# Gate columns copied sooner, chunk 2 spread ahead of chunk 0's values, output gates and weight splits in another order, in a linear-attention and gated-feed-forward kernel on one core

## What is computed

```python
for t in range(S):
    m_new = np.maximum(f_gate[:, :, t] + m, i_gate[:, :, t])
    f_stab = np.exp(f_gate[:, :, t] + m - m_new)
    i_stab = np.exp(i_gate[:, :, t] - m_new)
    m = m_new
    C = f_stab[:, :, None, None] * C + i_stab[:, :, None, None] * np.einsum('bhd,bhe->bhde', vt, kt)
    n = f_stab[:, :, None] * n + i_stab[:, :, None] * kt
    denom = np.maximum(np.abs(np.einsum('bhd,bhd->bh', n, qt)), 1.0)[:, :, None]
    y[:, :, t] = sigmoid(o_gate[:, :, t]) * np.einsum('bhde,bhe->bhd', C, qt) / denom
x = (sigmoid(x @ w_gate) * (x @ w_val)) @ w_out
x = ((x @ w_a) * (x @ w_b)) @ w_out2
```

## Time and profile before

| | |
|---|---|
| median of the runs | 471.15 us |
| the profiled execution's own time | 470.95 us |
| its span | 468.9 us |
| PE busy | 458.4 us (98%), 2527 matmuls |
| DVE, ACT, POOL busy | 190.2, 197.4, 114.4 us |
| granted TensorE clock | 1.00 of full speed over the whole span |
| transfers | 37.42 MB, mean 80 GB/s |

### The profile page before, as it was taken

One profiled execution on the slowest core, in us unless ns is written; L12 is line 12 of the kernel. 1 busy time (PEld: TensorE's weight loads), 2 busy tenths in 40 slices (PEclk: granted clock), 3 DMA queues, 4 the chain that ended last, 5 costly groups with the idle time before them and its releaser, 6 DMA issues.

```text
span 468.9 us, 6630 instructions
## 1 busy us (share of the span) xinstructions
PE 458.4 (98%) x2527; PEld 403.5 (86%) x2527; DVE 190.2 (41%) x352; ACT 197.4 (42%) x360; POOL 114.4 (24%) x110
## 2 busy tenths in 40 slices
PE   8898999999999999999999999999999999999997
PEld 5787898898989898888888888888888888888886
DVE  7866346546564636334222243222232222322223
ACT  5863829574573828224344352222222222222222
POOL 4487746664032020002444541000000000000000
PEclk9999999999999999999999999999999999999999
DMA  5886764842524362000333200000010000100001
GB/s 146 226 240 197 235 192 131 251 130 75 159 83 125 113 183 93 1 2 0 100 122 111 98 0 1 0 2 0 1 56 1 0 1 0 58 0 1 0 1 56
DMA packets 21449, 37.42 MB, mean 80 GB/s; under 512 B 2835, under 2 KB 15670, under 8 KB 21418
## 3 DMA queue, kind: packets, MB, share of 16 engines
q1 hardware_dynamic: 21050, 35.94, 24.9%
q10 hardware_dynamic: 208, 0.71, 0.5%
q0 software_dynamic: 160, 0.35, 0.3%
HBM read 34.91 MB, written 2.04 MB: 79 GB/s over the span
## 4 chain that ended last, share of the span: by engine, by line
PE 92%; POOL 3%; DMA 2%; DVE 1%; SPq 1%; issue 1%; ACT 0%; POOLq 0%
PE bank L573 54%; PE bank L590 27%; PE bank L497 3%; PE bank L472 2%; DMA q_blk<-kq_in 2%; PE bank L488 1%; PE bank L463 1%; DMA vk<-vk_in 1%; PE bank L553 1%; POOL w_lo L1109 1%; PE bank L523 1%; PE bank L511 1%; POOL w_lo_mid L1109 0%; POOL w_lo_end L1109 0%; PE bank L435 0%
## 5 line engine op out<-in xcount | busy, mean ns | idle before, releaser
L944 DVE TENSOR_TENSOR h_ff<-bank,s_ff 128x512 f32<-128x512 f32 x72 | 49.7, 691 | 175.5 <-PE bank L573 175.2
L573 PE MATMUL bank<-xt,w_hi 128*128 128x512 f32 x360 | 118.6, 394 | 0.5 <-issue 0.5
L742 ACT CAST h_hi<-h_ff 128x512 fp32r<-128x512 f32 x72 | 44.6, 619 | 130.2 <-DVE h_ff L944 127.1
L735 ACT ACTIVATE s_ff<-bank 128x512 f32<-128x512 f32 x72 | 43.1, 598 | 124.1 <-PE bank L573 123.7
L573 PE MATMUL bank<-xt,w_lo 128*128 128x512 f32 x216 | 84.5, 391 | 0.0
L573 PEld LDWEIGHTS bank<-xt,w_hi 128*128 128x128 f32 x360 | 65.6, 188 | 12.3 <-issue 0.9
L950 DVE TENSOR_TENSOR h_lo<-h_ff,h_hi 128x512 fp32r<-128x512 f32 x72 | 52.5, 728 | 55.1 <-ACT h_hi L742 55.1
L573 PE MATMUL bank<-xt,w_hi_mid 128*128 128x512 f32 x180 | 59.3, 394 | 0.0
L573 PE MATMUL bank<-xt,w_hi_end 128*128 128x512 f32 x180 | 59.1, 393 | 0.0
L573 PEld LDWEIGHTS bank<-xt,w_lo 128*128 128x128 f32 x216 | 40.6, 188 | 8.8
L590 PE MATMUL bank<-w_hi,h_hi 128*128 128x320 f32 x144 | 45.1, 313 | 0.0
(11 more groups left out here) (125 smaller groups left out, 678.6 us busy)
## 6 DMA issues: line engine op xcount, KB each, us to landing
w_raw<-w_in SPq DMA_DIRECT2D x24, 544.0 KB, 3.8
vk<-vk_in SPq DMA_DIRECT2D x12, 344.0 KB, 3.6
levels<-a_scratch SPq DMA_DIRECT2D x7, 512.0 KB
k_both<-kq_in SPq DMA_DIRECT2D x18, 120.0 KB
q_blk<-kq_in SPq DMA_DIRECT2D x18, 120.0 KB
y<-rows_t SPq DMA_DIRECT2D x12, 160.0 KB, 1.9
q<-kq_in SPq DMA_DIRECT2D x10, 180.0 KB
osig_b<-o_in SPq DMA_DIRECT2D x8, 160.0 KB, 3.2
```

Of the source, the lines that this page charges most:

```text
L573: mm = pe.matmul(up_bank(u, gv)[:, :], w_part(low, f, (gv * 3 + kt) * P, P), xt[:, xb * TOK + g * TG:xb * TOK + (g + 1) * TG], start=(j == ...
L735: act.activation(s_ff[u % 2][:, :], up_bank(u, 0)[:, :], ACT.Sigmoid if u < UNITS // 2 else ACT.Copy).then_inc(act_s, 1)
L742: act.copy(h_hi[u % 2][:, :], h_ff[u % 2][:, :]).then_inc(act_h, 1)
L944: dve.tensor_tensor(h_ff[u % 2][:, :], up_bank(u, 1)[:, :], s_ff[u % 2][:, :], ALU.mult).then_inc(dve_h, 1)
```

## The change

On PE, chunk 2's spread goes ahead of chunk 0's values, the gate columns of chunks 2 and 3 are transposed before the second half of chunk 0's scores, and turn(3) goes ahead of to_state(3). ACT copies these columns between the two halves of chunk 0's weights, issues the load of osig_a one half later, and computes its sigmoid behind all of i_rows. SP loads the values of chunks 0 and 1 behind the rows of chunk 1, and chunk 2's queries ahead of the store of i_rows. POOL weighs chunk 1's values and makes low_rows before it issues chunk 3's transfers; it splits the first 384 columns of tile 0 (before: 768) ahead of open_x(3), and the rest ahead of the decays; up(0, 1) waits for that rest. Tiles 2, 5, 6, 9 and 10 are split earlier in their units, or in earlier units.

```diff
-        PARTS = ((0, 1, bank[3]), (1, 2, XY[0]), (2, CHUNKS, bank[2]))
+        PARTS = ((0, 1, bank[3]), (1, 2, bank[3]), (2, CHUNKS, bank[2]))
...
 (SP)        load_rows(0)
-            load_v(0)
             sp.wait_ge(tri_set1, 1)
             load_rows(1)
+            load_v(0)
+            load_v(1)
             sp.wait_ge(dve_split, 4)
             load_rows(2)
+            load_q(2)
             sp.wait_ge(act_irow, 1)
             store_rows(f_row, i_dram, 1, 2, st_irow)
-            load_q(2)
-            load_v(1)
...
 (PE: scores)
-                    wait(pe, act_cols, 2 if half else 0)
+                    wait(pe, act_cols, 4 if half else 0)
...
 (PE: up)
+                if u == 0 and gv:
+                    pe.wait_ge(pool_wlo, 1)
...
 (PE)        columns(0, 0, dve_gate, 5)
-            scores(0, 1)
             columns(0, 1, dve_rows, 1)
             pe.wait_ge(pool_sel, 5)
             spread(0)
+            pe.wait_ge(act_cols, 2)
+            columns(1, 0, dve_gate, 9)
+            columns(1, 1, dve_rows, 2)
+            scores(0, 1)
             scores(1, 0)
             scores(1, 1)
             spread(1)
-            pe.wait_ge(act_e, 1)
-            columns(1, 0, dve_gate, 9)
-            columns(1, 1, dve_rows, 2)
+            spread(2)
             values(0)
             to_state(0)
-            spread(2)
...
             scores(4, 0)
+            turn(3)
             to_state(3)
-            turn(3)
             scores(4, 1)
...
 (ACT)       weigh(0, 0)
+            gate_cols(1)
             weigh(0, 1)
+            weigh(1, 0)
             act.dma_start(osig_a[:, :], o_in[:, 0:ALONE * DM]).then_inc(ld_oa, 16)
-            weigh(1, 0)
             weigh(1, 1)
-            gate_cols(1)
-            act.wait_ge(ld_oa, 16)
-            act.activation(osig_a[:, :], osig_a[:, :], ACT.Sigmoid).then_inc(act_o, 1)
             act.wait_ge(act_cols, 3)
             weigh(2, 0)
             weigh(2, 1)
             for c in range(2, CHUNKS):
                 i_rows(c)
+            act.wait_ge(ld_oa, 16)
+            act.activation(osig_a[:, :], osig_a[:, :], ACT.Sigmoid).then_inc(act_o, 1)
             weigh(3, 0)
...
-            W_AT = {0: (2,), 1: (3, 4), 3: (5,), 4: (6, 7), 6: (8, 9), 7: (10, 11)}
+            W_EARLY = {0: (2,), 3: (5, 6), 6: (9, 10)}
+            W_AT = {1: (3, 4), 4: (7, 8), 7: (11,)}
...
                 gate(u)
+                for f in W_EARLY.get(u, ()):
+                    w_high(f)
...
 (POOL: w_low)
-                at = W1C if j == 0 else 0
+                at = W1C // 2 if j == 0 else 0
...
             weigh_v(0)
+            weigh_v(1)
+            (low_rows: a memset and four affine_selects, moved here)
             pool.wait_ge(pe_s, 4)
             (four dma_starts of chunk 3's keys and queries)
-            weigh_v(1)
...
             pool.wait_ge(act_whi, 1)
-            pool.tensor_tensor(w_part(1, 0, 0, W1C), w_raw[0][:, 0:W1C], w_part(0, 0, 0, W1C).bitcast(F32), ...)
+            pool.tensor_tensor(w_part(1, 0, 0, W1C // 2), w_raw[0][:, 0:W1C // 2], ...)
             open_x(3)
+            w_low(0)
             pool.wait_ge(act_dec, 1)
             decay(2)
             decay(3)
-            w_low(0)
             scale_q(4)
             pool.wait_ge(act_cols, 6)
             weigh_v(4)
             w_low(1)
-            (low_rows)
-            W_AT = {0: (2,), 1: (3, 4), 3: (5,), 4: (6, 7), 6: (8, 9), 7: (10, 11)}
+            w_low(2)
+            W_EARLY = {3: (5, 6), 6: (9, 10)}
+            W_AT = {1: (3,), 2: (4,), 4: (7,), 5: (8,), 7: (11,)}
...
                         weigh_v(n)
+                for f in W_EARLY.get(u, ()):
+                    w_low(f)
                 if k == 1 and last_with_state(n):
                     decay(n)
```

More of the change, by code:

```diff
@@ L1141, in _ @@
             weigh_v(0)
+            weigh_v(1)
+            pool.memset(low_rows[:, :], 1.0).then_inc(pool_low, 1)
+            pool.wait_ge(pool_low, 1)
+            for x in range(2):
+                pool.affine_select(low_rows[:, x:x + 1], low_rows[:, x:x + 1], [[0, 1]], ALU.is_gt, 0.0,
+                                   base=1 - (x + 1) * HD, channel_multiplier=1).then_inc(pool_low, 1)
+            pool.wait_ge(pool_low, 3)
+            for x in range(2):
+                pool.affine_select(low_rows[:, x:x + 1], low_rows[:, x:x + 1], [[0, 1]], ALU.is_gt, 0.0,
+                                   base=(x + 2) * HD, channel_multiplier=-1).then_inc(pool_low, 1)
             pool.wait_ge(pe_s, 4)
@@ L1157, in _ @@
             pool.wait_ge(act_whi, 1)
-            pool.tensor_tensor(w_part(1, 0, 0, W1C), w_raw[0][:, 0:W1C], w_part(0, 0, 0, W1C).bitcast(F32),
-                               ALU.subtract).then_inc(pool_wup, 1)
+            pool.tensor_tensor(w_part(1, 0, 0, W1C // 2), w_raw[0][:, 0:W1C // 2],
+                               w_part(0, 0, 0, W1C // 2).bitcast(F32), ALU.subtract).then_inc(pool_wup, 1)
             open_x(3)
+            w_low(0)
             pool.wait_ge(act_dec, 1)
@@ L1168, in _ @@
             w_low(1)
-            pool.memset(low_rows[:, :], 1.0).then_inc(pool_low, 1)
-            pool.wait_ge(pool_low, 1)
-            for x in range(2):
-                pool.affine_select(low_rows[:, x:x + 1], low_rows[:, x:x + 1], [[0, 1]], ALU.is_gt, 0.0,
-                                   base=1 - (x + 1) * HD, channel_multiplier=1).then_inc(pool_low, 1)
-            pool.wait_ge(pool_low, 3)
-            for x in range(2):
-                pool.affine_select(low_rows[:, x:x + 1], low_rows[:, x:x + 1], [[0, 1]], ALU.is_gt, 0.0,
-                                   base=(x + 2) * HD, channel_multiplier=-1).then_inc(pool_low, 1)
-            W_AT = {0: (2,), 1: (3, 4), 3: (5,), 4: (6, 7), 6: (8, 9), 7: (10, 11)}
+            w_low(2)
+            W_EARLY = {3: (5, 6), 6: (9, 10)}
+            W_AT = {1: (3,), 2: (4,), 4: (7,), 5: (8,), 7: (11,)}
             for u in range(3 * (NCH - ALONE) - 1):
```

## The result

The changed kernel takes 468.66 us (median of 20 runs, 467.60 to 477.68), the kernel before 472.70 (20 runs beside them, 470.74 to 480.57). The ratio of comparable runs is 0.9940 with a 95% interval of 0.9917 to 0.9963: a gain that can be measured, inside 2%. The profiled execution has a span of 466.1 us (its time 467.95) against 468.9: 2.8 us won, where the working forecast 3.55. Runs of one kernel differ by up to 10 us, a good part of it with the mean granted clock of TensorE, so beside the ratios I set the spans, and the runs with a mean clock of at least 0.999 ("clocked runs": 467.60 to 471.68 us for the changed kernel, so they too spread), against each other.

What follows compares the result with a forecast made beforehand. PE bounds the kernel, busy 458.45 of 468.90 us, with 5.92 us of waits as the ceiling. Gains of 0.8 + 1.9 + 0.85 = 3.55 us take 471.15 to 467.6 us; 8 in 10: 466.0 to 470.1.

Steps and rivals of the forecast that it cites:

- the front: Everything up to the first up-projection: gate columns, spread(2), loads, sigmoid, turn(3); start at 33.5 instead of 34.26, 0.8 us won.
- the signs put down: Expected in the trace: scores(2,0) near 14.5, wait before spread(3) at 20.5, up-projection 33.5, turn(4) 44.2, turn(6) 87.
- sign of being wrong: A wait over a microsecond behind the first up-projection, or that up-projection starting outside 32.3 to 35 us.
- the landing of chunk 3's rows: Before spread(3): last row issued at 17.2 us, landing taken as 3.3 us, so spread(3) at 20.5, 0.5 us won.
- rival B: Row loads land in 2.1 us, spread(3) waits for nothing else, turn(6) is fully covered: 466.4 us; chance 0.15.
- Rival C: Transfers eat the front: chunk 3's rows land at 22.1 or later, losing 1.1 to 1.3 us: 469.3; chance 0.20.
- Turn(4): PE's 1.99 us wait before turn(4) goes but for 0.1, as POOL splits tile 2 without idle: 1.9 us won.
- Turn(6): PE's 1.04 us wait before turn(6) shrinks, as POOL's splits of tiles 9 and 10 start earlier: 0.85 us won.
- rival D: At unit 6 tile 10 lands after 81.1 us and delays turn(6), making the kernel slower than before; chance 0.05.
- Free items: Small moves priced at nothing, among them gate_cols, the wait of up(0,1), and POOL's transfers behind weigh_v(1) and low_rows.
- rival E: Small new waits, at state_sum(2) or x_n behind longer POOL work, eat most of the gain: 470.4 us; chance 0.08.
- parts 2 and 3: The gains at turn(4), 1.9 us, and at turn(6), 0.85 us, from earlier low_rows and weight splits.

Runs made afterwards that it cites:

- Experiment 5: Changed kernel with osig_a's load issued earlier again and ACT's sigmoid of it back between chunks 1 and 2; ratio 0.9965 to the kernel before.
- 12: Second execution of the changed kernel with later chunks' i_rows moved on ACT from ahead of the sigmoid to behind x_high(0); 468.69 us, span 466.7.
- Experiment 3: Changed kernel with DVE's `sign` moved from ahead of the feed-forward loop to behind state(0), where POOL runs no split; ratio 0.9913 to the kernel before.
- 11: Kernel before with only low_rows made early on POOL, behind weigh_v(1), and `sign` left in place; ratio 0.9988 to the kernel before.
- experiment 9: Changed kernel with `sign` early behind state(0) and tile 10 split later in unit 6; ratio 0.9890 to the kernel before.
- Experiment 4: Changed kernel with tile 10 copied by ACT at the end of unit 6 and split by POOL behind open_x(6); ratio 0.9908 to the kernel before.
- experiment 6: Changed kernel with SP's loads back in the order of the kernel before, POOL's order as changed; ratio 1.0023 to the kernel before.
- kernel 10: Changed kernel with SP's loads in the old order and POOL's weigh_v(1) back behind chunk 3's transfers; ratio 0.9988 to the kernel before.
- kernel 1: Changed kernel with its front kept but low_rows, weight splits and the wait of up(0, 1) as before; ratio 0.9997 to the kernel before.
- kernel 8: Changed kernel with `sign` early, tile 10 split later and later chunks' i_rows moved behind x_high(0); ratio 0.9890 to the kernel before.

## Why the prediction was right, step by step

The time (467.6 forecast, 468.66 median, 467.95 in the profiled execution) and the bound were right: the gain is PE's idle time under a ceiling of 5.92 us, 2.8 us of it where the sum has 3.55. The sizes were off in opposite directions, the front 0.58 us better and the two turns together 1.38 us worse; that the total came this close is partly luck. Of the signs put down, scores(2,0) came as told (14.62, no wait) and neither sign of being wrong appeared; but spread(3) came at 19.00 instead of 20.5, with no wait of 1 to 2 us, and the waits before turn(4) and turn(6) are over 0.3. (A slip in the sum: 33.5 + 10.67 is 44.17, not 44.15.)

**The front: +0.8 forecast, +1.38 measured.** Issues came within 0.6 us of the working. The term that was mis-sized is the landing of chunk 3's rows: from 16.63 to spread(3) at 19.00 is at most 2.4 us, where I took 3.3; the bound from below, 2.1, was nearer. That was rival B's first half. Rival C, that the rows wait behind 344 KB of values, did not occur, but the rule cited for it was not put to the test: POOL had the values of chunk 1 at 10.46, 6 us before these rows were issued. Experiment 5 has rows issued half a microsecond behind 640 KB; they reached PE 4.0 us after issue (9.20 to 13.24), where in the changed kernel they took at most 2.5 (8.88 to spread(2) by 11.4). That is the direction of C, though not a proof of the rule. But spread(3) 2 us sooner brought only 1.4 at the up-projection, because ACT binds from there, as forecast: exp at 21.38 (forecast 20.9; 21.55 before), DVE's product of chunk 3 waits 1.76 us for it, and turn(1) waits 0.31 us for DVE and starts at 25.32, 1.39 us sooner than before (26.71). Experiment 5 prices the sigmoid's move at 0.6 to 0.9; 12 shows that ACT alone made sooner gives nothing, because the rows then set spread(3). The reverse, the rows alone sooner, was not run. The exp table cost 1.28 us and its neighbours followed at once (20.09 + 1.28 = 21.37), in agreement with the row, not with the 2.66 us of the Trainium skill (ScalarE: Activation LUTs, "What ACT_TABLE_LOAD costs").

**Turn(4): +1.9 forecast, +0.92 beyond the front.** The step that failed is "w_low(2) follows w_low(1) without idle: 39.1 + 2.5 + decay 0.76 + x_n 1.43 = 43.8". POOL did its part: its two splits ended at 41.08, where the sum has 41.6. Not in the sum was DVE. I had `sign` down as waiting for low_rows; with low_rows early it has its input, and then takes 2.47 us beside POOL's split, not 0.16. That, and h_low(0) held by the second split, made combine(4) late (x_raw at 42.18), POOL idle for 0.94 and the decay 1.19 instead of 0.76. By an estimate in the forecast's own terms POOL would have ended at 41.08 + 0.76 + 1.43 = 43.3 without them, and PE came at 43.85: no wait. Experiment 3, which moves `sign` and nothing else, takes the wait away; 11 shows the same hold on `sign` with nothing but low_rows moved. How much is lost is a matter of timing (experiment 9). The row was there to be read: `sign` of the kernel before took 0.70 us for 240 numbers.

**Turn(6): +0.85 forecast, +0.45.** Tile 10 was issued at 75.91 and reached ACT at 80.97, inside the 79.7 to 81.2 of rival D, just under the 81.1 from which it decides. ACT waited 1.12 us for it all the same with h_high(6) behind it, and h_low(6) met POOL's split of tile 10 and took 2.49 us. Experiment 4 gives the 0.47 back. But D's own sum does not give the wait: 80.97 + 5.8 = 86.8, and PE came at 87.38. x_n was done at 87.79, one microsecond later than that sum, because the decay took 1.20 us instead of 0.76 and POOL then waited 0.57 us for x_raw, which DVE made late. The step that failed is of the same kind as at turn(4): "Now w_low(9) and (10) go ahead of decay(6)" is priced on POOL alone. Whether tile 10's landing or the second split put h_low(6) where it is held, experiment 4 leaves open.

**Free items.** The wait of up(0, 1), gate_cols(0) and (1), and the five small instructions of low_rows cost PE nothing by themselves: none of them is named in PE's waits. That weigh_v(1) ahead of POOL's transfers costs nothing holds only with load_v(1) early, as the forecast assumed without saying so (experiment 6: 7.88 us of POOL). Nearest in kind was rival E, something small that eats into parts 2 and 3, for 1.4 us (2.75 forecast, 1.37 measured) and not 2.8; but of the causes it names neither was it, state_sum(2) nor longer work on POOL.

## What to carry to other kernels

When work is moved ahead on one engine, walk the queue of the engine beside it too, instruction by instruction: many of those on DVE that only read and write SBUF last until the POOL instruction that they meet is done. A tiny DVE instruction that takes 0.7 or 2.5 us is the mark of it; put it where POOL is idle, and look which instruction meets the split in its stead. When a load is moved, name what in any engine's in-order queue is placed behind its consumer.

## What the runs showed of the hardware

**POOL holds DVE.** A 120x2 tensor_scalar took 0.16 us alone and 2.47 and 2.48 us beside POOL's 2.6 us splits; the 128x512 h_low 0.69 us alone and 1.72, 2.42 and 2.49 us beside them; h_ff, which reads PSUM, took 0.68 us right between two held ones. Each ended a little behind POOL's instruction, by about what it takes alone or less: `sign` 0.03 us behind it in both cases (0.16 alone), h_low 0.54 to 0.56 (0.69 alone). So they look as if they had done nothing until POOL was nearly or quite done. It works the other way too: the 120x328 decay took 1.19 us where h_low was still at work as it began, and 0.74 in experiment 3, and the split behind h_low(0) in experiment 3 took 2.99 us. Not every SBUF instruction is held: the reciprocal of 128x8 took 0.20 us in the middle of that split (39.32, experiment 3). The Trainium skill (SBUF — State Buffer, "SBUF: two separate sides") says that of a POOL instruction and a DVE instruction that needs the shared ports (one with two SBUF inputs, or in a two-port mode) the second is blocked until the first is done; for h_low and the decay, with two SBUF inputs each, these rows agree. That `sign`, with one input, ran in such a mode no row shows; that it was held the rows do.

**The clock falls in some executions and not in others.** The granted clock was 0.50 (1.2 GHz of 2.4) for 20.5 us from within a wait of 6.07 us (kernel 6), for 6.8 us behind one of 1.89 (kernel 10), and, in kernel 1, for

```profile
46.90:50.30 3.40, 3.40 (x13) 3.01 (x12) 0.91 (x3) 1.79 (x2) 2.52 (x2) 0.50 0.89 247
```

beginning 1.3 us after the end of its wait of 2.05 us before turn(4). A long wait is not needed for it, and does not always bring it. In kernel 8 PE had waited no more than 0.64 us at a time since its first scores (5.64), and had

```profile
29.00:32.40 3.40, 3.40 (x13) 2.79 (x12) 1.84 (x6) 2.06 (x8) 2.53 (x4) 0.50 0.87 253
```

while the kernel before waited 1.99 us before turn(4) and ran at a mean of 1.00 in its profiled execution. Beside the experiments 12 of 20, 10 of 29 and 10 of 23 of its runs were clocked ones. What decides it was not settled. It is part of the reason that the medians spread more than the terms that are argued about here; the rest, up to 4 us between clocked runs, was not looked into.
